# Low parts of the first weights on TensorE, products placed behind chunk 0's solves, and the last stores by accumulator, in a delta-rule kernel with two feed-forward layers

## The reference

```python
# attention: B, H, S, D = 4, 8, 768, 48
k_n = k / (norm(k) + 1e-06)
for t in range(S):
    y[:, :, t] = einsum('bhd,bhde->bhe', q[:, :, t], state)
    v_old = einsum('bhde,bhd->bhe', state, kt)
    state = state + bt * einsum('bhd,bhe->bhde', kt, vt - v_old)
# then twice, on x of shape (3072, 384), d_ff = 2048
h = x @ w_in
g = piecewise(h)        # layer 1: h if h >= 1, 0 if h <= -1, else (h + 1)^2 / 4; layer 2: max(h, 0)^2
x = g @ w_out
```

## Time and profile before

| | us |
|---|---|
| median of 3 runs | 1012.62 |
| lowest and highest | 1011.58, 1012.86 |
| the profiled execution | 1011.66 |
| its span | 1008.5 |
| PE busy | 966.4 |
| DVE busy | 593.7 |
| ACT busy | 411.6 |

### The profile page before, as it was taken

One profiled execution on the slowest core, in us unless ns is written; L12 is line 12 of the kernel. 1 busy time (PEld: TensorE's weight loads), 2 busy tenths in 40 slices (PEclk: granted clock), 3 DMA queues, 4 the chain that ended last, 5 costly groups with the idle time before them and its releaser, 6 DMA issues.

```text
span 1008.5 us, 24126 instructions
## 1 busy us (share of the span) xinstructions
PE 966.4 (96%) x10400; PEld 796.3 (79%) x10400; DVE 593.7 (59%) x1118; ACT 411.6 (41%) x728; POOL 9.5 (1%) x17
## 2 busy tenths in 40 slices
PE   4379999999999999999999999999999999999997
PEld 4268788888888888888888888888888888888886
DVE  6888978786877677768635774433434334333332
ACT  4458544433433344443435554323333233332332
POOL 1000000000000000000000000000000000000000
PEclk7589999999999999999999999999999999999999
DMA  7143133003200320020003511001010010000000
GB/s 234 44 138 106 59 98 101 9 18 85 83 10 19 93 75 11 20 70 32 3 13 107 176 63 63 1 1 63 1 63 1 1 63 1 31 1 1 32 1 31
DMA packets 28376, 50.91 MB, mean 50 GB/s; under 512 B 2288, under 2 KB 15728, under 8 KB 28272
## 3 DMA queue, kind: packets, MB, share of 16 engines
q1 hardware_dynamic: 28272, 49.39, 15.3%
HBM read 39.94 MB, written 9.44 MB: 49 GB/s over the span
## 4 chain that ended last, share of the span: by engine, by line
PE 92%; DVE 5%; issue 1%; ACT 1%; DMA 0%; ACTq 0%; DVEq 0%
PE psum L966 39%; PE psum L942 38%; PE psum L795 2%; PE psum L838 2%; PE psum L773 2%; PE psum L818 2%; PE psum L809 2%; DVE tmp L1066 1%; DVE x_inv L1069 1%; PE psum L894 1%; PE psum L866 1%; PE psum L871 1%; PE psum L879 1%; PE psum L751 1%; PE psum L734 1%
## 5 line engine op out<-in xcount | busy, mean ns | idle before, releaser
L966 PE MATMUL psum<-g_hi,w 128*128 128x512 f32 x1152 | 392.1, 395 | 0.0
L942 PE MATMUL psum<-x_hi,w 128*128 128x512 f32 x1152 | 386.6, 390 | 1.2 <-DVE x_lo L1166 1.2
L1184 DVE TENSOR_TENSOR g_lo<-act_g,g_hi 128x512 fp32r<-128x512 f32 x192 | 132.6, 691 | 210.7 <-ACT g_hi L650 210.7
L966 PEld LDWEIGHTS psum<-g_hi,w 128*128 128x128 f32 x1152 | 216.2, 188 | 50.7 <-issue 2.0
L942 PEld LDWEIGHTS psum<-x_hi,w 128*128 128x128 f32 x1152 | 216.2, 188 | 46.8 <-issue 1.4
L650 ACT ACTIVATE g_hi<-act_g 128x512 fp32r<-128x512 f32 x192 | 121.4, 632 | 273.4 <-PE psum L966 238.8
L966 PE MATMUL psum<-g_lo,w 128*128 128x512 f32 x576 | 224.6, 390 | 0.0
L942 PE MATMUL psum<-x_lo,w 128*128 128x512 f32 x576 | 224.1, 389 | 0.0
L1178 DVE TENSOR_TENSOR act_g<-act_g 128x512 f32<-128x512 f32 x96 | 66.4, 692 | 112.9 <-ACT act_g L643 112.9
L942 PEld LDWEIGHTS psum<-x_lo,w 128*128 128x128 f32 x576 | 108.1, 188 | 22.1
L966 PEld LDWEIGHTS psum<-g_lo,w 128*128 128x128 f32 x576 | 108.2, 188 | 20.6
(11 more groups left out here) (83 smaller groups left out, 568.9 us busy)
## 6 DMA issues: line engine op xcount, KB each, us to landing
kt_sb<-in_k_t SPq DMA_DIRECT2D x24, 256.0 KB, 4.2
qt_sb<-in_q_t SPq DMA_DIRECT2D x24, 256.0 KB, 3.6
kn_sb<-in_k_n SPq DMA_DIRECT2D x20, 256.0 KB, 4.0
ring<-in_v_s SPq DMA_DIRECT2D x24, 192.0 KB, 2.8
between_layers<-y_out SPq DMA_DIRECT2D x6, 768.0 KB, 4.0
x_sb<-between_layers SPq DMA_DIRECT2D x6, 768.0 KB, 5.6
result<-y_out SPq DMA_DIRECT2D x6, 768.0 KB, 3.9
wi_st<-in_w_in SPq DMA_DIRECT2D x7, 384.0 KB, 3.9
```

The source lines that it names most:

```text
L942: ins = pe.matmul(h_ps[n % 2][:, :], w_in_part(layer, f // GW, part)[:, kt, fs], x[:, kt, :], start=(kt == 0 and j == 0), stop=(kt == KT - ...
L966: ins = pe.matmul(acc[kt][:, :], w_out_part(layer, f // GW, part)[:, f % GW, ds], g[n % 2][:, :], start=(f == 0 and j == 0), stop=(f == NF ...
L1184: dve.tensor_tensor(g_lo[n % 2][:, :], act_g[n % 2][:, :], g_hi[n % 2][:, :].bitcast(F32), ALU.subtract).then_inc(g_lo_ready, 1)
```

## The change

- **ACT and PE, weights.** For groups 0, 1 and 2 the low part is no longer made by DVE. PE multiplies the staged weights by an identity (`eye`) and the high parts, read as float32, by a negative identity (`minus_eye`) into one PSUM bank, half a part (384 columns) at a time (`low_parts`), and ACT copies the bank to the low part (`low_out`). Two banks, 4 and 6, are used in turn. That makes 24 float32 matmuls of 384 columns and 12 copies. They need the grams' banks, so they come behind `gram_out`.
- **Order on ACT.** The splits of groups 0 and 1 with their low parts go ahead of `gd_out`; group 2 goes behind the first eight scalings; the other 24 scalings follow behind group 2. `solved` of block 0 takes three of the four copies.
- **Order on PE.** The diagonals of chunk 1 wait for the low parts of groups 0 and 1, `solve(0)` for those of group 2. `keys_by_queries(k)` goes directly behind `solve(k)`, for all four. Behind each `substitute` stands one product of 256 columns into a spare bank whose result nobody reads (`keep_busy`), and one of 512 columns behind `gram_of(B)`.
- **DVE.** Six low parts are gone; `masked` is placed after the new order.
- **Loads.** Weight groups 0 and 1 are issued ahead of the keys of chunk 1, group 2 behind them and thus ahead of the queries, of two row blocks of values and of group 3.
- **End.** `last_products` runs the last two steps' second products accumulator by accumulator, six matmuls each; ACT copies each accumulator when it is done, and SP stores it with a DMA of its own.

```diff
+        low_ps = bank[4], bank[6]
...
             sp.dma_start(beta_b[:, :, :], beta).then_inc(beta_loaded, 16)
             load_v(0)
+            load_weights(0, 0, w_in1, w_out1)
+            load_weights(0, 1, w_in1, w_out1)
             for m in range(B, 2 * B):
                 load_kt(m)
-            for m in range(QUERIES):
-                load_qt(m)
-            load_weights(0, 0, w_in1, w_out1)
-            for k in range(1, RING):
-                load_v(k)
-            load_weights(0, 1, w_in1, w_out1)
+            load_v(1)
+            load_weights(0, 2, w_in1, w_out1)
+            load_qt(0)
+            load_v(2)
+            load_v(3)
+            load_qt(1)
+            load_qt(2)
+            load_weights(0, EARLY, w_in1, w_out1)
...
-                store_out(t)
-            sp.wait_ge(out_stored, 32 * NTT)
+                if t < NTT - 1:
+                    store_out(t)
+            for kt in range(KT):
+                sp.wait_ge(acc_ready, KT * (2 * NTT - 1) + kt + 1)
+                sp.dma_start(out.rearrange("(k p) (t j) -> t p k j", p=P, j=TT)[NTT - 1][:, kt, :], y_out[:, kt, :]
+                             ).then_inc(out_stored, 16)
...
+            def low_out(g, out_part):
+
+                for half_of in range(2):
+                    act.wait_ge(low_done, 4 * g + 2 * out_part + half_of + 1)
+                    act.activation(flat_part(g, LOW, out_part, half_of), low_ps[half_of][:, 0:GW * DM // 2], ACT.Copy
+                                   ).then_inc(w_lo_ready if half_of else low_half, 1)
...
+            split_weights(0, 0, 0)
+            split_weights(0, 0, 1)
+            low_out(0, 0)
+            low_out(0, 1)
+            split_weights(0, 1, 0)
+            split_weights(0, 1, 1)
+            low_out(1, 0)
+            low_out(1, 1)
             for hp in range(2):
                 gd_out(1, hp)
+            scaled_first(0)
+            split_weights(0, 2, 0)
+            split_weights(0, 2, 1)
+            low_out(2, 0)
+            low_out(2, 1)
+            for k in range(1, NB):
+                scaled_first(k)
             for k in range(NB):
-                scaled_first(k)
-            for g in range(2):
-                split_weights(0, g, 0)
-                split_weights(0, g, 1)
-            for k in range(NB):
-                solved(k, 0)
-                solved(k, 1)
+                for b in range(3 if k == 0 else 2):
+                    solved(k, b)
                 if k == 0:
                     gain_root(1)
-            split_weights(0, 2, 0)
-            split_weights(0, 2, 1)
...
                 if n == 1:
-                    pe.wait_ge(gram_ready, 2 * B)
-                    pe.wait_ge(gd0_ready, NB * B)
+                    pe.wait_ge(low_half, 4)
+                    pe.wait_ge(w_lo_ready, 4)
...
                 else:
-                    pe.wait_ge(scaled0, H)
-                    pe.wait_ge(gd_ready, 2)
+                    pe.wait_ge(w_lo_ready, 2 * EARLY)
...
+            def low_parts(g, out_part):
+
+                at, turn = stage_of(0, g)
+                pe.wait_ge(eye_ready, 4)
+                pe.wait_ge(ws_loaded[at], 32 * turn)
+                pe.wait_ge(w_hi_ready, 2 * g + out_part + 1)
+                pe.wait_ge(gram_ready, 2 * B)
+                pe.wait_ge(gd0_ready, NB * B)
+                if g == 2:
+                    pe.wait_ge(gd_ready, 2)
+                for half_of in range(2):
+                    wait(pe, w_lo_ready if half_of else low_half, 2 * g + out_part)
+                    out_ps = low_ps[half_of][:, 0:GW * DM // 2]
+                    whole_part = staged(0, g)[out_part].rearrange("p a c -> p (a c)")
+                    pe.matmul(out_ps, eye[:, :], whole_part[:, half_of * GW * DM // 2:(half_of + 1) * GW * DM // 2],
+                              start=True, stop=False)
+                    pe.matmul(out_ps, minus_eye[:, :], flat_part(g, HIGH, out_part, half_of).bitcast(F32),
+                              start=False, stop=True).then_inc(low_done, 1)
...
+            def last_products():
+
+                pe.wait_ge(g_hi_ready, 2 * STEPS)
+                pe.wait_ge(g_lo_ready, 2 * STEPS)
+                acc = acc_of(1, NTT - 1)
+                for kt in range(KT):
+                    ds = slice(kt * P, (kt + 1) * P)
+                    for n in range(2 * STEPS - 2, 2 * STEPS):
+                        for j, (part, g) in enumerate(((HIGH, g_hi), (HIGH, g_lo), (LOW, g_hi))):
+                            ins = pe.matmul(acc[kt][:, :], w_out_part(1, n % NF // GW, part)[:, n % NF % GW, ds], g[n % 2][:, :],
+                                            start=False, stop=(n == 2 * STEPS - 1 and j == 2))
+                    ins.then_inc(tail_done, 1)
...
             for b in range(B):
                 first_grams_of(b)
+            for g in range(2):
+                low_parts(g, 0)
+                low_parts(g, 1)
             for hp in range(2):
                 diagonals_of(1, hp)
-            for m in range(B - 1):
-                keys_by_queries(m)
+            low_parts(2, 0)
+            low_parts(2, 1)
+            pe.wait_ge(mask_ready, 2)
             for k in range(NB):
                 solve(k)
-                if k == 2:
-                    keys_by_queries(B - 1)
+                keys_by_queries(k)
                 if k < NB - 1:
                     substitute(k + 1)
+                    keep_busy(2 * P, bank[4])
             for m in range(B):
                 outputs(m)
             gram_of(B)
+            keep_busy(4 * P, bank[1])
...
                 if k == 2:
-                    split_weights(0, 0, 0)
-                if k == 3:
                     masked(1)
-                solved_first(k, 2)
+                if k:
+                    solved_first(k, 2)
                 solved_first(k, 3)
...
-            masked(2)
-            split_weights(0, 1, 0)
-            split_weights(0, 1, 1)
             masked(B - 1)
-            split_weights(0, 2, 0)
-            split_weights(0, 2, 1)
             x_low(0, 0)
```

## The result

| | before | after |
|---|---|---|
| median | 1012.74 (1011.58 to 1014.17, 4 runs) | 1023.91 (1020.57 to 1027.25, 4 runs) |
| ratio, 95% interval | 1 | 1.011, 1.0073 to 1.0146 |
| profiled execution | 1011.66 | 1023.06 |
| its span, and the time outside it | 1008.5, 3.2 | 1021.3, 1.8 |
| F, start of the first product of layer 1 | 68.43 | 81.66 |

A forecast was written before the change was run, and what follows sets the result against it. PE was taken as the bound, so a shift of layer 1's first product shifts the end: +4.1 us there and -0.2 at the end make +3.9 on 1011.66, giving 1015.6; range 1010.5 to 1020.

The forecast's parts named there:

- The identity products: Low parts on PE: 24 float32 products of 384 columns, 1.23 us each at 1.2 GHz, 0.66 at 2.4 GHz.
- C: Rival, far slower: low-part products never raise PE's clock, first product of layer 1 near 92, time 1035; chance 0.08.
- D: Rival, faster: an identity product costs 0.17 us like an fp32r one, time 1006.7; chance 0.09.
- The diagonals, "two times 1.29": PE's diagonals of chunk 1, waiting for low parts of groups 0 and 1: 32.4 to 35.0 us.
- "Loads ... Cost nothing": SP's reordered loads: some 3 MB behind group 2, there by 36 us, not needed before 38, so no cost.
- The chain ACT, PE, ACT, PE behind the diagonals: Group 2's copies, eight scalings, high part and identity products: from 35.0 to the last low copy's end at 45.6 us.
- 24 scalings between L and the copies of the first solve: On ACT behind the last low copy: 5.5 us, ending at 51.1, delaying the first solve's copies to 52.6.
- From L to F: From the last low copy at 45.6 us, through scalings, solves and outputs, to layer 1's first product at 72.5.
- the 1.0 us for a cold start of the steps: Added because PE, idle ahead of `substitute(1)`, runs it and the next solve at 1.2 GHz.
- Rival A: The forecast itself, with clock changes moved a few microseconds: first product of layer 1 at 71.3 to 76.2, 1013.7 to 1020.0; chance 0.66.
- The end: Last two steps' products, copies and stores: PE idles 1.5 us, yet a gain of 0.2, bounds 0.9 gained, 0.5 lost.
- The base: Sum made against the profiled execution, 1011.66 us, with 68.43 to layer 1's first product and 3.2 outside the span.

The follow-up runs named there:

- scalings_early: Changed kernel with all 32 scalings on ACT ahead of `gd_out`, where ACT waits for PE; 1019.26 us, ratio 1.0077.
- after_again: The changed kernel, unaltered, executed and profiled once more; 1025.85 us in one run.
- burst_ahead: Changed kernel with 768 KB more of loads directly behind the load of weight group 2; 1026.03 us in one run.
- shifted: Changed kernel with 32 more products of the same shape ahead of the diagonals of chunk 1, on their own line; 1027.55 us in one run.
- loads_first: Changed kernel with the load of weight group 2 put back behind the small loads that need no wait; 1022.38 us, ratio 1.0101.
- more_spare: Reworked version of the change (loads reordered, low parts in other banks, scalings between low copies, split end) with more spare products around substitutions; 1008.89 us, ratio 0.9962.
- behind_only: Kernel before with only the products of keys and queries put behind each solve, no spare products, low parts on DVE; 1014.70 us, ratio 1.0022.
- both_moved: Changed kernel with the edits of `loads_first` and `scalings_early` together; 1018.18 us, ratio 1.0047.

## Why the prediction was wrong

Point by point, in the order of its steps; times of the profiled execution after.

- **The identity products: right.** I took L871's price, 1.23 and 0.66 us a product. By the starts of L939, one pair apart, a pair takes 2.56 at 1.2 GHz (19.19 and 21.75) and 1.29 at 2.4 GHz (52.36 and 53.65), so a product takes 1.28 and 0.645. The first starts at 17.78, forecast 17.4; the clock rises near 23.1, forecast 22.3; groups 0 and 1 are done at 32.56, forecast 31.7. Rivals C and D are out; by the formula of the Trainium skill, page "TensorE: Matmul & The Clock Gate", section "Back-to-back issue gap", a product would have taken an estimated 0.16 warm, and the trace shows four times that.
- **The diagonals, "two times 1.29": this step failed.** They took 10.83 us instead of 2.6: two holes of 5.50 and 1.59, and 1.1 us because 127 records behind the first hole ran at 1.2 GHz. With the 1.0 us by which they started later, their end is 44.22 instead of 35.0. The row is from the middle of the kernel, 88.52; the row of the same line in the prologue has a hole of 2.09 in it (21.41 us), and I did not take it. What stands in the place of the step: PE waits for its own instructions at the records 216 and 343, a wait that the sum put at nothing.
- **"Loads ... Cost nothing": in doubt with it.** I asked only who needs the data (they were there by about 38, forecast 36) and not what else uses the DMA engines. PE's instructions do. With the loads out of the way the holes are 2.1 instead of 7.1 in one pair of executions and 3.3 instead of 5.9 in the mean over kernels. So of the 8.2 us some 3 to 5 go with the loads and the rest is the price of small products by the hundred; how the loads act on the length stays open.
- **The chain ACT, PE, ACT, PE behind the diagonals: right.** From their end to L, the end of the last low copy, I had 10.6 us and it is 10.8 (44.22 to 54.98).
- **24 scalings between L and the copies of the first solve: right.** 5.50 by the row, forecast 5.5; PE idle 4.76 with ACT's `u_sb` as cause, forecast over 3. The trace of `scalings_early` has them away from there, with 5.9 us less of waiting on PE.
- **From L to F: the size right, one term by luck.** 26.7 against 26.9. Warm steps are 4.16 apart, forecast 4.1 to 4.3. But the 1.0 us for a cold start of the steps is only one draw: in `after_again`, `burst_ahead`, `shifted` and `loads_first` the stretch is 3.5 us longer. Rival A's F up to 76.2, 3.7 above the forecast, would just have covered that.
- **The end: nearly right.** Idle PE 1.60, forecast 1.5 (in that sum 1000.33 and 4.1 make 1004.4, 0.1 less than I wrote); the store takes 2.4 us from the end of the last copy (1018.89 to 1021.3), forecast 3.2; the span gains 0.5, forecast 0.2 with bounds -0.5 to 0.9. Outside the span it is 1.8 us instead of 3.2. With the old end it was near 2.0 in about two thirds of all runs and 2.9 to 3.6 in the others, and the profiled execution of before was one of the latter; with the change's end it was 1.7 to 1.8 in every run. So most of these 1.4 us are that execution's luck, and 0.2 to 0.3 are a gain of the new end over the usual 2.0. I left this time as it was.
- **The base.** F was 68.43 in the one execution that I had. With 940.1 behind it and 2.0 outside the span, the median of before, 1012.6, belongs to an F of about 70.5; the unchanged start gave 69.27 to 71.08 in later kernels. The low F and the long time outside the span offset each other in my sum.

Together: F was forecast 72.5 and is 81.66, 9.2 late, of which 8.2 are the diagonals (7.1 of holes and 1.1 of clock) and 1.0 the earlier small delays; the time outside the span takes 1.4 of it back, the end 0.3, and 1023.06 stands against 1015.6. My range ended at 1020.0 because it was built from the clock alone: nothing in it stood for a stretch in which PE waits for none of the others.

## What to carry to other kernels

Before moving hundreds of small instructions onto the path, look for idle time with "issue" as its cause in the rows of the same line at the same place of the program, not in the tidiest row of that line; where such a hole is covered before, ask what it costs uncovered. And when loads are reordered, count the DMA engines as a resource of the instruction supply too: with the loads that nobody waits for moved away, the holes were shorter by 2.7 us in the mean, though not in every pair of kernels. An order that pays only at the upper clock must be priced at both levels, since one program showed both.

## What the runs showed of the hardware

- **PE waits for its own instructions.** The holes stand at a count (behind 216 records from the start, then 127 further, with their weight loads), not at a place; `shifted` and `more_spare` show it. With the DMA engines at a share of 0.07 or less they last 0.3 to 2.8 us, at 0.48 or more 0.3 to 5.5 us. The two ranges overlap, and 3.23 us came at a share of 0.20 (`behind_only`).
- **A busy PE may stay at 1.2 GHz.** 17.7 us without idle time at 0.51 in `loads_first`, with products of 32 to 96 rows and a spare product of 128 rows and 256 columns per step; while the identity products, which read 128 rows, came to 2.4 GHz in every kernel that has them, 2.7 us (47.66 to 50.35) to 5.3 us (17.78 to 23.1) after their first in the profile after.
- **"issue" has a second meaning.** In the changed kernel the first product of group 1, at 27.32, has 1.46 us of idle time with "issue" ahead of it. That is no hole in the supply: it is 1.46 again in `loads_first` and `both_moved`, because ACT's high part of group 1 (26.28, 0.83 us) ends just ahead of it. What tells the two apart is that the length of a supply hole changes from run to run, and that its place goes with the count of records.
